# Narrow opening blocks, a slice order that runs to and fro, a trimmed first tile and the leaky step on ScalarE, in an attention and two-FFN kernel

## The reference

```python
# 1: causal window attention with sinks
scores = q @ k.T / sqrt(D)
keep = (pos_k < 4) | ((0 <= pos_q - pos_k) & (pos_q - pos_k < 128))
a = softmax(where(keep, scores, -1e9));  x = a @ v      # (1536, 512)
# 2: h = x @ w_in (512, 2048);  g = max(0.01 * h, h);  x = g @ w_out (2048, 512)
# 3: h = x @ w_in2;             g = h * sigmoid(h);    y = g @ w_out2
```

## Time and profile before

| What | Value |
|---|---|
| time, median of 3 runs | 679.76 us (678.94 to 679.97) |
| the profiled execution, its span | 677.8 us |
| PE busy | 634.3 us, 94% |
| DVE busy | 415.4 us, 61% |
| ACT busy | 362.4 us, 53% |
| POOL busy | 99.3 us, 15% |
| mean granted TensorE clock | 0.980 |

### The profile page before, as it was taken

How to read it: one execution, slowest core, us unless ns; L and a number is a source line. 1 busy time by engine, 2 the same in 40 slices (tenths; PEclk the granted TensorE clock), 3 DMA queues, 4 the chain that set the end, 5 groups by cost and what they waited for, 6 DMA issues and landing times.

```text
span 677.8 us, 9233 instructions
## 1 busy us (share of the span) xinstructions
PE 634.3 (94%) x3048; PEld 529.2 (78%) x3048; DVE 415.4 (61%) x894; ACT 362.4 (53%) x788; POOL 99.3 (15%) x133
## 2 busy tenths in 40 slices
PE   2566799999999999999999999999999999999997
PEld 2565678888887778888888888888888888888886
DVE  7999977888888887886654545333343333433332
ACT  4667766666667666664544446443344434443342
POOL 5544422222324232200000000000000000000000
PEclk9977799999999999999999999999999999999999
DMA  6343981211121120000222221000010000100001
GB/s 145 110 113 111 297 261 34 47 48 33 48 47 33 48 63 17 1 1 1 93 94 93 94 94 31 1 0 1 1 62 1 0 1 1 58 6 0 1 1 62
DMA packets 12334, 36.50 MB, mean 54 GB/s; under 512 B 2048, under 2 KB 2048, under 8 KB 12288
## 3 DMA queue, kind: packets, MB, share of 16 engines
q1 hardware_dynamic: 12288, 35.92, 18.1%
HBM read 32.77 MB, written 3.15 MB: 53 GB/s over the span
## 4 chain that ended last, share of the span: by engine, by line
PE 62%; DVE 22%; ACT 8%; issue 6%; DMA 1%; ACTq 0%; SPq 0%; DVEq 0%
PE y_ps L808 29%; PE h_ps L781 29%; DVE sm L515 4%; DVE prob L597 4%; DVE pT L524 3%; DVE g_f L559 3%; ACT g L428 2%; ACT g_f L417 2%; DVE g L569 2%; DVE x L537 2%; DVE psT L529 1%; DVE row_inv L590 1%; PE o_ps L748 1%; ACT prob L355 1%; ACT win L400 1%
## 5 line engine op out<-in xcount | busy, mean ns | idle before, releaser
L781 PE MATMUL h_ps<-x,win 128*128 128x512 f32 x1152 | 284.0, 391 | 0.5 <-DVE win L544 0.5
L781 PEld LDWEIGHTS h_ps<-x,win 128*128 128x128 f32 x1152 | 212.8, 188 | 42.6 <-DVE win L544 0.8
L808 PE MATMUL y_ps<-g,wout 128*128 128x512 f32 x576 | 145.7, 393 | 0.0
L808 PE MATMUL y_ps<-wout,g 128*128 128x512 f32 x576 | 138.2, 389 | 0.0
L569 DVE TENSOR_TENSOR g<-g_f,g 128x512 fp32r<-128x512 f32 x96 | 70.9, 739 | 91.7 <-ACT g L421 85.4
L551 DVE TENSOR_TENSOR wout<-w_raw,wout 128x512 fp32r<-128x512 f32 x96 | 72.4, 754 | 86.9 <-ACT wout L408 86.7
L808 PEld LDWEIGHTS y_ps<-wout,g 128*128 128x128 f32 x576 | 108.1, 188 | 22.5
L808 PEld LDWEIGHTS y_ps<-g,wout 128*128 128x128 f32 x576 | 103.9, 188 | 18.6
L408 ACT ACTIVATE wout<-w_raw 128x512 fp32r<-128x512 f32 x96 | 60.2, 627 | 90.9 <-PE y_ps L808 90.9
L355 ACT ACTIVATE prob<-sm,neg_max 128x260 f32<-128x260 f32 x96 | 48.7, 508 | 43.3 <-DVE neg_max L515 42.7
L419 ACT ACTIVATE g_f<-h_ps 128x512 f32<-128x512 f32 x48 | 28.7, 598 | 69.3 <-PE h_ps L781 69.3
(11 more groups left out here) (72 smaller groups left out, 507.2 us busy)
## 6 DMA issues: line engine op xcount, KB each, us to landing
w_raw<-w SPq DMA_DIRECT2D x32, 512.0 KB, 3.5
qk_raw<-qk SPq DMA_DIRECT2D x48, 260.0 KB, 4.2
v_raw<-vt SPq DMA_DIRECT2D x12, 256.0 KB, 2.6
y<-qk_raw SPq DMA_DIRECT2D x12, 256.0 KB, 2.2
vs_raw<-vsink SPq DMA_DIRECT2D x8, 8.0 KB, 3.5
```

Of the source, the lines that this page charges most:

```text
L781: ins = mm(h_ps[:, :], win[:, F % 2, wp, c * P:(c + 1) * P], x[:, xp, c, i * BLK:(i + 1) * BLK], start=(c == 0 and wp == HI and xp == HI), ...
L808: ins = mm(y_ps[d][:, :], a[:, d * P:(d + 1) * P], r, start=(f == 0 and wp == HI and gp == HI), stop=(f == FT - 1 and wp == LO))
```

## The change

1. **Blocks.** Layer one works on four blocks, two of 256 tokens and two of 512. It has 64 steps F (32 narrow, 32 wide) in place of 48; layer two keeps its 48. A narrow step is the same 24 matmuls over 256 columns. Narrow steps have two `h` buffers (`h_ps` and a free `y_ps` bank) and four places in `g`, so that PE runs two `hidden` ahead of a `project`. A narrow block's four outputs lie two to a bank.
2. **Start.** The head is 11 pairs (`FS`). `hidden(0)` and `hidden(1)` run in pair 10 and need the `x` of two tiles only. From pair 11 the narrow steps are woven in at 1, 1, 2 to a pair (32 steps over pairs 11 to 34), then one wide step per pair to `LAST`.
3. **Slices to and fro.** Even blocks go through the slices upward, odd blocks downward. The last 8 slices of a block stay split (`KEPT`) and are the first 8 of the next. 72 slices are split in place of 96. `w_raw` is a ring of 4 slices (`RING`); a slice is loaded when the one four ahead of it has been split.
4. **First tile of a batch.** `width(T)` is 128 for tiles 0 and 6: scores, minimum, exponential, scaling, transposes (2 for 4), their split and the weighing (3 matmuls for 6) take the own slot only. Tiles with `T % 6 < 2` do no sink work. Their sinks are plain columns of the own slot or of the slot before, and the mask changes accordingly.
5. **Leaky on ScalarE.** ACT reads `h` twice through Prelu with slope 0.01, once into `g_f32` and once into `g`, as layer two does with Silu; the copy, DVE's `scalar_tensor_tensor` and the rounding copy are gone.
6. **Smaller.** The low part of the transposed sinks is one DVE instruction over 64 rows in place of two over 32. Three DVE memsets go. `stack_sink_values` and its 8 loads move from the start to pairs 5 and 3. The loads of the first four slices are issued in iterations 1 to 4.

```diff
+    WIDE, NARROW = 512, 256
+    BLOCKS = (
+        ((0, NARROW), (NARROW, NARROW), (WIDE, WIDE), (2 * WIDE, WIDE)),
+        tuple((i * WIDE, WIDE) for i in range(NB)),
+    )
+    KEPT = 8
+    RING = 4
+    steps = [(layer, b, FT - 1 - i if b % 2 else i)
+             for layer in (0, 1) for b in range(len(BLOCKS[layer])) for i in range(FT)]
...
+        if F % FT < FT - KEPT or b == len(BLOCKS[layer]) - 1:
+            del resident[layer, f]
+            free.append((split_slot[j], F))
...
+    FS = 11
+    for a in range(FS, LAST):
+        n = (1, 1, 2)[(a - FS) % 3] if F < N_NARROW else 1
+        for _ in range(n):
+            ticks_of[a].append(F)
+            F += 1
...
+    made_in, made = {-1: [0, 1]}, 2
+    for F in range(NSTEP):
+        lead = 0 if F == FT - 1 else 2 if F + 2 < N_NARROW else 1
+        made_in[F] = list(range(made, min(F + lead, NSTEP - 1) + 1))
+        made += len(made_in[F])
+    for j, s in enumerate(first_step):
+        was, was_out = at, at_out
+        start, i = s - s % FT, s % FT
+        if s < FT:
+            at, at_out = s - 4, s - 3
+        elif i < FT - KEPT:
+            at = at_out = s - 6
+        else:
+            i -= FT - KEPT
+            at = start + 2 + i + i // 2
+            at_out = at + 1
...
+        def h_of(F):
+            if is_wide(F):
+                return h_ps[:, :]
+            return (h_ps if F % 2 == 0 else y_ps[3] if F < FT else y_ps[1])[:, 0:NARROW]
...
+            for a in range(LAST):
+                T, j = divmod(a, PAIRS)
+                if T + 1 < TILES:
+                    if j == 0:
+                        load_qk(T + 1, 0)
+                    if j == 2:
+                        load_qk(T + 1, 1)
+                        load_v(T + 1)
+                if a == 3:
...
+                if 1 <= a <= RING:
+                    load_w(a - 1)
...
             def take_hidden(F):
+                func, slope = (ACT.Prelu, 0.01) if F < N_L0 else (ACT.Silu, 0.0)
                 act.wait_ge(h_done, F + 1)
+                wait(act, g_ready, F - g_slots(F) + 1)
+                nc.scalar.activation(g_f32[:, g_at(F)], h_of(F), func, alpha=slope)
+                wait(act, y_done, F - g_slots(F) + 1)
+                nc.scalar.activation(g[:, 0, g_at(F)], h_of(F), func, alpha=slope).then_inc(h_taken, 1)
...
-            def leaky(F):
-                if F >= NF:
-                    return
-                dve.wait_ge(h_taken, F + 1)
-                a = g_f32[:, F % 2, :]
-                nc.vector.scalar_tensor_tensor(out=a, in0=a, scalar=0.01, in1=a, op0=ALU.mult,
-                                               op1=ALU.max).then_inc(leaky_done, 1)
...
                 for part in (HI, LO):
-                    ins = mm(bank_[:, 0:PAN], q_st[:, h, :], k_hl[:, part, h, :], start=part == HI, stop=part == LO)
+                    ins = mm(bank_[:, 0:W], q_st[:, h, :], k_hl[:, part, h, 0:W], start=part == HI, stop=part == LO)
...
+                ticks = ticks_of[a]
+                ahead = made_in[ticks[0]] if ticks and ticks[0] != FT else []
+                for G in ahead[:1]:
+                    hidden(G, 0)
+                if not head and a < NPAIR:
+                    scores(2 * a + 1)
+                for n, G in enumerate(ahead):
+                    if n:
+                        hidden(G, 0)
+                    hidden(G, 1)
+                if a in sinks_of:
+                    transposes("sinks", sinks_of[a])
+                if head and 1 <= a:
+                    transposes("pair", a - 1)
+                if 2 <= a <= NPAIR + 1:
+                    weigh_values(a - 2)
+                if ticks:
+                    project(ticks[0], 0)
+                if not head and a <= NPAIR:
+                    transposes("pair", a - 1)
...
+                for F in ticks[1:]:
+                    for G in made_in[F]:
+                        hidden(G, 0)
+                        hidden(G, 1)
                     project(F, 0)
+                    project(F, 1)
```

More of the change, by code:

```diff
@@ new lines, in sink_window_attention_two_ffn @@
+    N_L0 = FT * len(BLOCKS[0])
+    N_NARROW = 2 * FT
+    split_of, split_w, split_slot, slot_left, first_step = [], [], [], [], []
+    resident, free = {}, [(s, -1) for s in range(KEPT)]
+    for F, (layer, b, f) in enumerate(steps):
+        if (layer, f) not in resident:
+            slot, left = free.pop(0)
+            resident[layer, f] = len(split_w)
+            split_w.append((layer, f))
+            split_slot.append(slot)
+            slot_left.append(left)
+            first_step.append(F)
+        j = resident[layer, f]
+        split_of.append(j)
+        if F % FT < FT - KEPT or b == len(BLOCKS[layer]) - 1:
+            del resident[layer, f]
+            free.append((split_slot[j], F))
@@ new lines, in has_sinks @@
+    def has_sinks(T):
+        return T % TPB >= 2
+    sink_pairs = [u for u in range(NPAIR) if has_sinks(u // PAIRS)]
+    sink_at = {u: i for i, u in enumerate(sink_pairs)}
+    sinks_of = {2 * e + 3: e for e in range(NPAIR // 2) if has_sinks(e // 2)}
+    job = {}
+    for a in range(LAST):
+        if a in sinks_of:
+            job["sinks", sinks_of[a]] = len(job)
+        if 1 <= a <= NPAIR:
+            job["pair", a - 1] = len(job)
+    EARLY = next(a for a in range(LAST) if FT in ticks_of[a]) - 1
@@ L70, in sink_window_attention_two_ffn @@
+    N_EARLY = job["pair", EARLY - 2] + 1
+    E_EARLY = 2 * NARROW // P
+    S_FOUR, S_THREE = 2 * FS - 4, 2 * FS
     with ExitStack() as ctx:
@@ L173, in j_split @@
         def j_split(T):
[L174 to L184, removed]
+            return 1 if T < 3 else 2
+        split_1 = {(T, 3): T + 1 for T in range(2)}
+        split_1.update({(T, 0): T for T in range(3, TILES)})
+        CONSTS = 2 + 2 + 2 + 2 + 1 + 2
         def wait(eng, s, value):
@@ L225, in _ @@
                             sp.dma_start(vs_raw[r * n:(r + 1) * n, b, :], vsink[b]).then_inc(vs_loaded, 16)
[L226 to L253, removed]
+                if 1 <= a <= RING:
+                    load_w(a - 1)
+                if a < FS:
+                    load_ws(a - FS)
+                for F in ticks_of[a]:
+                    load_ws(F)
+            for F in REST:
+                load_ws(F)
+                i, f = divmod(F - N_L0, FT)
+                if i > 0 and f == 1:
+                    store(i - 1)
+            store(NB - 1)
             for t in range(TB):
@@ L745, in weigh_values @@
                     wait(pe, x_ready, freed(o_bank, e))
-                for s in range(2):
+                only = not has_sinks(T)
+                slots = (0,) if width(T) == P else (0, 1)
+                for s in slots:
                     for vp, pp in PASSES:
@@ L849, in _ @@
-            while F < 2 * NF:
-                hidden(F + 1, 0)
-                hidden(F + 1, 1)
+                        w_t, g_t = wout[:, split_slot[split_of[F]], wp, :], g[:, gp, g_at(F)]
+                        a, r = (w_t, g_t) if layer == 0 else (g_t, w_t)
+                        ins = mm(y_of(F, d), a[:, d * P:(d + 1) * P], r,
+                                 start=(first and wp == HI and gp == HI and (wide or d % 2 == 0)),
+                                 stop=(last and wp == LO), skip_group_check=not wide)
@@ L852, in _ @@
+            for F in REST:
+                for G in made_in[F]:
+                    hidden(G, 0)
+                    hidden(G, 1)
                 project(F, 0)
                 project(F, 1)
-                F += 1
 def kernel(**inputs):
```

550 lines of the change are left out of this document (263 added, 287 removed).

## The result

The changed kernel takes 688.12 us (median of 4 runs, 686.56 to 690.34), the kernel before 679.35. The ratio is 1.0131, 95% interval 1.011 to 1.0151: slower by 8.8 us, where I had forecast 666 and a gain. The profiled execution has a span of 688.4 us. It is the longest of the four, so its terms add up to some 2 us more than the median would.

A forecast was written before the change was run, and what follows sets the result against it. DVE was taken to bound the head, PE the woven stretch and the FFN alone. Span 677.8 - 37.0 + 19.5 + 2.0 - 3.7 + 1 + 1 + 4 = 664.6, median 1.96 above, so 666 us; range 652 to 678.

The forecast's parts named there:

- Start: End of the head: first hidden at 49 us (44 to 54) in place of 85.95, moving the start by 37.0 us.
- Narrow matmuls, weight loads, trimmed tiles: Layer one's 256-column matmuls at 116 ns, loads hidden: +2.0 us; lighter tiles 6 and 7: -3.7 us.
- Pairs 11 to 34: Narrow stretch: pairs 5.9 to 6.4 us apart, PE over 90% busy.
- 4 (DVE): Pairs 11 to 19: DVE's waits slow the pairs by +4 us, between nothing and +9.
- the forecast's three terms: Narrow stretch: -3.7 us for lighter tiles, +1 for one more block border, +4 for DVE.
- PE bounds it: Woven stretch of the kernel before: PE busy for 179.85 of 182.67 us, DVE for 152.61, so PE is the bound.
- Pairs 35 to 46: Stretch with one wide step a pair: pairs 7.6 us apart, as before.
- edit at nothing: Leaky step on ScalarE, like the 24 splits saved, lies under PE's work and was priced at no gain.
- DVE takes over as the bound: Rival, chance 0.15: start at 54 (+5), DVE in pairs 11 to 19 (+5), other narrow pairs (+3); 679 us.
- the fast case: Rival, chance 0.15: start at 44 to 46, DVE hides, deeper hidden takes up PE's small stalls; 654 us.
- The rival of a clock below full: Rival, chance 0.05: DVE's waits drop the clock to 1.2 GHz for a third of the narrow stretch; 691 us.
- Tables: Rival, chance 0.05: Prelu and Exp on ACT reload activation tables in turn, 2.57 us a woven pair; 701 us.

The follow-up runs named there:

- e7: Changed kernel with DVE's two splits of a slice cut to 64 of 512 columns from the ninth slice on; 686.43 us.
- e13: Changed kernel with one matmul pass of three in the narrow steps only (256 narrow matmuls in place of 768); 678.21 us.
- e3: Changed kernel with the leaky step back on DVE and its copy and rounding copy on ScalarE; 707.15 us.
- e11: e4 with the leaky step back on DVE and its two copies on ACT; 670.94 us.
- e8: Changed kernel with GpSimd's low parts of q and k cut to 8 columns a head from tile 3 on; 680.77 us.
- e9: Changed kernel with ACT's q and k copies moved ahead of the next pair's first exponential from pair 11 on; 684.56 us.
- e4: Changed kernel without narrow blocks and early start: layer one on three blocks of 512, first hidden in pair 19; 666.45 us.
- e5: Changed kernel with DVE's queue reordered: wout and some win splits one step later, last low_g behind the next first minimum; 696.81 us.
- e10: e9 with a pair's last win copy also ahead of the next first exponential, its DVE split behind the next first minimum; 698.37 us.

## Why the prediction was wrong

The sum said 664.6 for the span; the profile has 688.4. By its terms:

- **Start.** 49 forecast, 51.93 measured: +2.9, within its bounds. From there to pair 11's first minimum passed 7.14 us, at a granted clock of 0.65; the kernel before took 7.33 (85.95 to 93.28), and I had added 1 for the clock, which was not needed.
- **Narrow matmuls, weight loads, trimmed tiles.** The price of 116 ns held (0.87 us for six).
- **Pairs 11 to 34: the step that failed.** I had 24 x 5.9 - 3.7 (lighter tiles) + 1 (border) + 4 (DVE) = 142.9 us. It took 165.95, +23: nearly the whole error of 23.8. I wrote "DVE needs 5.8 us a pair. PE needs ... 5.9. They are level", and took the larger of two amounts of work, averaged over three pairs. Two things were wrong in this. First, the bound is neither amount but the length of the way through the in-order queues. DVE's amount came out as I had it: 50.06 us busy in pairs 11 to 19 (5.6 a pair, forecast 5.8) and 67.98 in pairs 20 to 34 (4.5, forecast 4.8). Yet the pairs came 6.92 us apart in the first part and 6.91 in the second, where I had let PE alone set the pace. e7 took DVE's work away and e13 PE's, and neither gave back the loss; e3 and e11, and e8 by way of DVE's durations, changed the way's length, and the time followed. Second, the average hides that the pairs are uneven. By my prices a pair with one step has 24 x 0.116 + 2.17 = 4.95 us, and it takes 5.81 (from 4.5 in tile 6 to 7.0). A pair with two has 7.74 and takes 8.23. 15 x 0.86 + 7 x 0.49 = 16.3 us are lost so. The two pairs with a block border, 23 and 34, take 10.57 and 10.68 us, 8.6 more than these prices, where I had added 1. PE was busy for 8.76 and 9.09 us of them, in the first at a granted clock of 0.84, and pair 34 also takes in the first `hidden` of 512 columns, 2.91 us. What else makes the borders long was not tested. Together that is 24.9 us, of which the forecast's three terms had 1.3; the rest is rounding.
- **"PE bounds it" in the kernel before** was half the truth. PE was 98% busy and the chain ran through DVE and ACT, so two bounds of nearly one length stood there. PE was idle there for 2.8 of 182.67 us, so the ring cost the kernel before next to nothing. A wide step had covered it with 5.44 us of matmuls. Halve the columns of a step, and the ring, which does not get shorter by half, stands open. The chain of waits for that stretch would have told.
- **Pairs 35 to 46.** 7.29 in place of 7.61: -3.8. e11 shows that the leaky step's place is worth 4.5 us in a wide version, so it was no "edit at nothing": I had costed it by ACT's and DVE's busy time, and not by the waits that it adds.
- **The rival "DVE takes over as the bound"** named the right stretch and the wrong mechanism, with a price of +13, of which 8 in the stretch that lost 23. I gave "a narrow step leaves less PE time between scores and the transposes that need the softmax" as a remark against the fast case and never priced it. The loss is of that kind.
- **The rival of a clock below full** was not it either. The granted clock of pairs 11 to 34 was 0.97. In e9's profile it was 1.00 there, and the pairs still came 6.68 us apart.
- **Tables.** There was no reload. ACT's groups by line and shape in the changed kernel, over the whole span, have these two table loads and no more, though readings of `h` by Prelu stand between exponentials:

```profile
L447 ACT ACT_TABLE_LOAD x1 | 1.3, 1283 | 0.7 <-PEq L936 0.7
L492 ACT ACT_TABLE_LOAD x1 | 1.3, 1283 | 0.0
```

  The rule for kernel authors in the Trainium skill ("ScalarE: Activation LUTs") that relu and max belong on VectorE is not borne out here; the leaky step on ScalarE gains 4.5 us in the wide version and, with the move of two copies that e3 also makes, 19 in the narrow one. The measurement decides.

The rest of e4's 13.2 us fits the prediction's rows: its pair 20 begins at 87.8 where the kernel before had it at 93.3 (5.5 us of head work), and 3.7 us of PE work in tiles 6 and 7. That split was not tested alone, and the first part overlaps the leaky step's 4.5 by 1.1 (in e11 pair 20 begins at 88.9). Left open is also which single way through the ring sets each pair, and whether some order of the queues would let the narrow version run at PE's 5.9 us; e5 and e10 show only that work put between the two minima costs. Narrow blocks with the steps spread evenly over the pairs were not tried, nor narrow blocks without the early start.

## What to carry to other kernels

Before the work that covers a chain is halved, ask for the chain of waits of that very stretch, not only for busy shares: an engine can be 98% busy while a ring through the other engines' in-order queues is as long as its work, and then a change that shortens its steps can lay the ring open. Sum the larger bound pair by pair and not over the average of unequal pairs. When a second buffer removes a wait and the time stays, the wait was where the ring showed; look at what the next wait is.

## What the runs showed of the hardware that was not expected

DVE instructions lengthen beside POOL's: `low_g` over 256 columns took 1.52 us at 69.11 beside a POOL subtraction of 1.63, and 0.43 at 162.59. With POOL's low parts of q and k cut short (e8) POOL was busy for 19.48 us of the stretch in place of 43.87, DVE's instructions took 106.36 us in place of 118.06, and the kernel was 7.3 us faster, though POOL was 26% busy there and never the bound. And with a third of the narrow matmuls (e13) PE was busy for 106.72 of 158.88 us at a granted clock of 0.83, where it had been 143.40 of 165.95 at 0.97: PE had 606 instructions there in place of 1099, but its busy time fell only by a quarter. The pairs with one step kept their 5.81 us even so.
